# Attention and feed-forward kernel: phi made by GpSimd alone, low parts of weights on VectorE, a new order of all engines

## The chip, the cores and the metric

The kernel runs on one core of one Trainium2 chip. The metric is the device time of one execution in microseconds, as the median of several runs. The engines of the core are called as the profile calls them: PE (TensorE; PEld are its weight loads), DVE (VectorE), ACT (ScalarE), POOL (GpSimd) and SP (SyncE, which here only issues DMAs).

## What is computed

There are 4 batches of 8 heads, 576 positions and head size 64. For each head

```python
scores = q @ k.T / 8, masked causally; a = softmax(scores); local = a @ v
phi(x) = where(x > 0, x, exp(x) - 1) + 1
mem_out = (phi(q) @ M_prev) / (phi(q) @ z_prev + 1e-6)
g = sigmoid(beta)                      # one per head
attn = g * mem_out + (1 - g) * local   # rows: 4 * 576 tokens, 512 columns
h = attn @ w_in1; y = where(h > 0, h, exp(min(h, 0)) - 1) @ w_out1
h = y @ w_in2;    out = (h * clip(h + 3, 0, 6) / 6) @ w_out2
```

The two layers have 512 inputs, 2048 hidden values and 512 outputs. All is float32. Note that phi(x) = max(x, 0) + exp(min(x, 0)), and also max(x + 1, min(exp(x), 1)).

## The kernel before

**Numbers in two parts.** Products that need float32 precision are made from a rounded part (fp32r, named hi) and the rest (lo): x times w is x_hi w_hi + x_hi w_lo + x_lo w_hi. So each tile is rounded by one engine and its low part is made as a subtraction by another.

**Attention.** Two heads form a pair, and there are 16 pairs, handled as a software pipeline: in each step every engine works on two or three pairs in a fixed order that is written out by hand. Queries are cut into four tiles of 128 rows (0 to 3) and a last tile of 64 rows that holds both heads (4). Score tiles are made in the order 4, 3, 2, 1, 0, in two PSUM places in turn, so that `scores` of one tile waits for the exps (`exp_done`) of the tile two before. DVE takes the row maximum (`max_rows`, L951, L955), and ACT the exp with its row sum (`exp_last`, `exp_rows`). PE then transposes the probabilities in chunks (`turn`: G, C00, C01, C10, C11, C2, C3), and also a small tile of row factors R and phi in two pieces (PHI, TAIL). All chunks go through a ring of two PSUM banks, which the product for the first 128 rows (Q0, made by `first_rows`) shares. A chunk is rounded by ACT (`round_chunk`, L731 to L750), its low part made by DVE (`split_chunk`, L962 to L976), and only then is its bank free for the chunk two places on. `first_values` and `times_v` multiply the chunks with v, `times_m` multiplies phi with M, ACT copies one half of the result aside (`low_rows`, `low_first`), and DVE adds the halves into x_all (`sum_x` L1005, `sum_first` L1012).

**phi and the factors.** GpSimd writes x + 1 into the tile phi (`phi_line`, L404), ACT writes exp(x) (`exp_q`, L758), and DVE joins the two (`phi_of_q`, L984). GpSimd multiplies phi with z (`phi_by_z`, L376), DVE sums this (`norms`, L989) and, after the last exp of the pair, makes the reciprocals of all denominators (`row_stats`, L994 to L999). GpSimd makes the row factors from them (`factors`, L386 to L390), scales phi (`scale_phi`, L396), and also scales q (L344), rounds v and M (`round_vm`) and makes their low parts (`low_vm`, L359, L360). The factors of the softmax are turned by PE, sent to DRAM by SP and read back spread over all partitions into r_rows (`spread_r`, L277 to L285), with which GpSimd multiplies the finished pair in x_all (`store_x`, L368).

**Queue of SP.** It issues in order and waits in order: for each step the spread of R, then (in three steps) two weight loads, then the loads of qk and nat (v, q, z and M of a pair) three pairs ahead. nat is released by `low_vm`, phi and `phi_by_z` of two pairs before.

**Feed-forward.** The 2304 tokens are six chunks of 384. A chunk takes 16 hidden tiles: `hidden` (L578, 12 matmuls) and two tiles later `output` (L591, 12 matmuls in the first layer; L599, 9 in the second). Between them, in the first layer, ACT makes the exp (L790) and DVE four operations (L1029, L1031, L1042, L1044); in the second, DVE makes five (L1035 to L1044). Weights come in 32 tiles of 128x1024, through four staging places: DMA, rounding by ACT (`hi_weights`, L695), low part by GpSimd (`lo_weights`, L339); `hidden` waits for this (`w_split`). Tiles 0 to 2 are made during attention. From tile 6 on the place of a tile lies over attention's buffers, so ACT waits for the last `store_x`. The first three groups `hidden` of chunk 0 are woven into the work of the last pair. Tiles of the second layer are made while the last chunk of the first runs, as their places become free, the last four after it.

## Time and profile before

| what | value |
|---|---|
| median of 3 runs | 1075.93 us (1075.89 to 1076.37) |
| the profiled execution, its own time | 1078.44 us |
| its span, first to last instruction | 1076.6 us |
| busy PE / PEld / DVE / ACT / POOL | 1037.4 / 921.7 / 696.7 / 306.1 / 228.5 us |
| mean granted clock of PE | 0.993 |
| moved by DMA | 49.34 MB, 46 GB/s |

The span has four parts. Attention runs from the start to about 258 us, the first layer's work begins at 258.42, the second layer's at about 668, and the rows of the last chunk are stored at the end. Matmuls overlap and their ends are modelled, so a busy share of PE says how long something was under way on it, not how much it could still take. A wait is put down to the instruction that released it last.

### The profile page before, as it was taken

What the parts mean: (1) busy time and instruction counts of PE and PEld (TensorE: products, weight loads), DVE (VectorE), ACT (ScalarE), POOL (GpSimd) and SP (SyncE); (2) the same over time, 40 slices, a digit from 0 to 9 for tenths busy, and PEclk for the clock granted to TensorE, in tenths of its full rate; (3) what the DMA queues carried; (4) which work ended last, traced back from release to release, by engine and by line L of the source; (5) the groups of instructions that cost most, each with busy time, mean ns of one, the idle gap of its engine ahead of it and who ended that gap; (6) DMA issues with size and microseconds to landing.
All of it is one profiled execution on the core that took longest, in us unless ns stands there. A gap on an engine that the chain in (4) does not pass through costs nothing.

```text
span 1076.6 us, 15983 instructions
## 1 busy us (share of the span) xinstructions
PE 1037.4 (96%) x5792; PEld 921.7 (86%) x5792; DVE 696.7 (65%) x1309; ACT 306.1 (28%) x737; POOL 228.5 (21%) x265
## 2 busy tenths in 40 slices
PE   6899999999899999999999999999999999999998
PEld 2666666667899999999999999899899999999997
DVE  4889888988975445454444587756556565565654
ACT  4877777777322121121211234001010010100100
POOL 4676565654640000000000055200000000000000
PEclk8999999999999999999999999999999999999999
DMA  6233532321330000000000033000000000000000
GB/s 235 96 109 117 167 125 98 117 76 40 124 114 1 1 1 0 0 0 0 0 0 0 0 124 109 1 1 30 0 22 7 0 29 0 29 0 0 29 0 30
DMA packets 22007, 49.34 MB, mean 46 GB/s; under 512 B 5184, under 2 KB 5328, under 8 KB 21968
## 3 DMA queue, kind: packets, MB, share of 16 engines
q1 hardware_dynamic: 21968, 48.85, 13.3%
q8 instruction: 21, 0.34, 0.1%
q14 instruction: 18, 0.15, 0.0%
HBM read 44.04 MB, written 4.79 MB: 45 GB/s over the span
## 4 chain that ended last, share of the span: by engine, by line
PE 79%; DVE 16%; ACT 3%; issue 1%; DMA 0%; POOL 0%; ACTq 0%; DVEq 0%
PE ps L578 36%; PE ps L599 19%; PE ps L591 18%; DVE phi L984 3%; DVE neg_max L955 2%; DVE pt_lo L965 2%; DVE x_all L1005 2%; PE ps L464 1%; DVE pt_lo L968 1%; PE ps L519 1%; DVE phi_t_lo L974 1%; PE ps L534 1%; DVE neg_max L951 1%; ACT pt_hi L744 1%; ACT phi_t_hi L748 1%
## 5 line engine op out<-in xcount | busy, mean ns | idle before, releaser
L578 PE MATMUL ps<-x_hi,w 128*128 128x384 f32 x1536 | 391.2, 335 | 0.0
L578 PEld LDWEIGHTS ps<-x_hi,w 128*128 128x128 f32 x1536 | 279.2, 188 | 7.3
L578 PE MATMUL ps<-x_lo,w 128*128 128x384 f32 x768 | 257.7, 336 | 0.0
L591 PE MATMUL ps<-h_hi,w 128*128 128x384 f32 x768 | 196.4, 336 | 4.9 <-DVE h_lo L1044 4.9
L599 PE MATMUL ps<-w,h_hi 128*128 128x512 f32 x576 | 180.3, 394 | 2.1 <-DVE h_lo L1044 2.1
L1042 DVE CAST h_hi<-act_tmp 128x384 fp32r<-128x384 f32 x192 | 109.1, 568 | 101.3 <-PE ps L591 52.5
L339 POOL TENSOR_TENSOR w<-stage,w 128x1024 f32 (+1 forms) x32 | 77.8, 2441 | 345.6 <-ACT w L695 345.6
L591 PEld LDWEIGHTS ps<-h_hi,w 128*128 128x128 f32 x768 | 139.3, 189 | 6.0 <-DVE h_lo L1044 5.9
L578 PEld LDWEIGHTS ps<-x_lo,w 128*128 128x128 f32 x768 | 144.1, 188 | 0.0
L790 ACT ACTIVATE e_act<-ps 128x384 f32<-128x384 f32 x96 | 47.3, 492 | 289.2 <-PE ps L578 289.2
L591 PE MATMUL ps<-h_lo,w 128*128 128x384 f32 x384 | 128.8, 336 | 0.0
L599 PEld LDWEIGHTS ps<-w,h_hi 128*128 128x128 f32 x576 | 107.6, 189 | 20.9 <-issue 2.4
L1044 DVE TENSOR_TENSOR h_lo<-act_tmp,h_hi 128x384 fp32r<-128x384 f32 x192 | 113.4, 591 | 6.7
L1035 DVE TENSOR_SCALAR act_tmp<-ps 128x384 f32<-128x384 f32 x96 | 53.4, 556 | 98.9 <-PE ps L578 98.9
L599 PE MATMUL ps<-w,h_lo 128*128 128x512 f32 x288 | 114.2, 397 | 0.0
L1029 DVE TENSOR_SCALAR act_tmp<-e_act 128x384 f32<-128x384 f32 x96 | 39.6, 413 | 112.7 <-ACT e_act L790 111.3
L767 ACT ACTIVATE x_hi<-x_all 128x384 fp32r (+1 forms) x48 | 21.2, 514 | 300.2 <-PE ps L578 300.2
L591 PEld LDWEIGHTS ps<-h_lo,w 128*128 128x128 f32 x384 | 72.6, 189 | 0.0
L712 ACT ACTIVATE prob<-ps,neg_max 128x512 f32<-128x512 f32 (+3 forms) x128 | 67.0, 526 | 10.7 <-DVE neg_max L955 10.2
L599 PEld LDWEIGHTS ps<-w,h_lo 128*128 128x128 f32 x288 | 54.4, 189 | 11.7
L464 PE MATMUL ps<-qk 64*128 64x512 f32 (+3 forms) x256 | 54.5, 504 | 4.8 <-ACT prob L712 4.8
L1039 DVE TENSOR_TENSOR act_tmp<-ps,act_tmp 128x384 f32<-128x384 f32 x96 | 53.5, 558 | 3.3
(117 smaller groups left out, 1167.7 us busy)
## 6 DMA issues: line engine op xcount, KB each, us to landing
nat<-nat_in SPq DMA_DIRECT2D x16, 768.0 KB, 6.3
qk<-qk_t SPq DMA_DIRECT2D x16, 608.0 KB, 3.9
stage<-w_in SPq DMA_DIRECT2D x32, 256.0 KB, 2.6
stage<-w_out SPq DMA_DIRECT2D x32, 256.0 KB, 2.9
out<-rows_out SPq DMA_DIRECT2D x18, 256.0 KB, 2.1
r_rows<-r_dram SPq DMA_DIRECT2D x32, 128.0 KB, 2.6
r_rows<-r_dram SPq DMA_DIRECT2D x32, 16.0 KB, 2.5
r_dram<-r_turned SPq DMA_DIRECT2D x16, 4.5 KB
```

Source lines behind the costliest of these rows:

```text
L339: pool.tensor_tensor(tile[:, 1], stage[:, r], tile.bitcast(F32)[:, 0], ALU.subtract).then_inc(w_split, 1)
L464: pe.matmul(ps[:, at:at + WIDTH[i]], qk[d, u, P * i:P * i + P], qk[d, u, QCOLS:QCOLS + WIDTH[i]], start=True, stop=False)
L578: mm = pe.matmul(ps[:, bank:bank + CHUNK], w[:, n, wp, 0, cols], xp[:, m, :], start=(m == 0 and part == 0), stop=(m == KM - 1 and part == 2))
L591: mm = pe.matmul(ps[:, Y_AT + 512 * m:Y_AT + 512 * m + CHUNK], w[:, n, wp, 1, cols], hp[:, n % 2, :], start=(n == 0 and part == 0), stop=( ...
L599: mm = pe.matmul(ps[:, Y_AT + 512 * m:Y_AT + 512 * m + DM], hp[:, n % 2, rows], w[:, n, wp, 1, :], start=(n == 0 and part == 0), stop=(n = ...
L712: act.activation(rows_of(u, i, a), ps[:, at:at + WIDTH[i]], ACT.Exp, bias=neg_max[:, u, x:x + 1], scale=-1.0, accum_out=stats[:, u, x:x + ...
L790: act.activation(e_act[:, n % 2, :], ps[:, 512 * (n % 4):512 * (n % 4) + CHUNK], ACT.Exp).then_inc(h_exp_done, 1)
L1029: dve.tensor_scalar(tmp, e_act[:, n % 2, :], 1.0, -1.0, ALU.min, ALU.add).then_inc(e_free, 1)
L1035: dve.tensor_scalar(tmp, h, 3.0, 0.0, ALU.add, ALU.max).then_inc(act_step, 1)
L1039: dve.tensor_tensor(tmp, h, tmp, ALU.mult).then_inc(h_free, 1)
L1042: dve.tensor_copy(h_hi[:, n % 2, :], tmp).then_inc(h_hi_done, 1)
L1044: dve.tensor_tensor(h_lo[:, n % 2, :], tmp, h_hi.bitcast(F32)[:, n % 2, :], ALU.subtract).then_inc(h_split, 1)
```

## The change

Six things change together.

1. phi is now max(x, 0) + exp(min(x, 0)). GpSimd makes min(x, 0) (`cut_q`), ACT its exp in place (`exp_q`), GpSimd max(x, 0) (`phi_line`) and the sum (`phi_sum`). DVE's `phi_of_q` is gone.
2. r_rows has two buffers, each with a semaphore of its own.
3. Weight tiles 3 to 31 get their low part from DVE, one after each tile of activations, in chunk 0 of the first layer, in its last chunk (from hidden tile 5), and in the first chunk of the second layer (the last five). Tiles 0 to 2 stay on GpSimd. DVE's loops over chunks are cut so that these chunks stand outside.
4. SP issues the first four weight loads one step at a time, behind nat, and the next three two steps apart.
5. ACT's rounding of weights 0 to 2 moves to steps 5 to 7, at the end of the step.
6. The order inside a step is new. With A the pair whose chunks are turned and B and C the next two, it is now:

- PE: C11, C2 of A; scores 1 of B; C3, times_v 1, PHI, times_v 2 of A; scores 0 of B; TAIL, times_v 3 and 4 of A; G of B; times_m of A; scores 4 of C; first_rows of A; C00 of B; scores 3 of C; C01, C10 of B; scores 2 of C; first_values 0, R, first_values 1 of B.
- ACT: exps 3 (head 0) of B; R of A; exps 3 (head 1) of B; C11, C2 of A; exps 2 (head 0) of B; C3 of A; exps 2 (head 1) and 1 (head 0) of B; PHI, TAIL of A; exps 1 (head 1) and 0 of B; G of B; low_rows, low_first of A; C00 of B; exp_q of C; exp_last of C; C01, C10 of B.
- DVE: row_stats, G of A; sum_x of the pair before A; maximum 4 of B; sum_first of the pair before A; C00 of A; maximum 3 of B; C01, C10 of A; maximum 2 of B; C11, C2 of A; maximum 1 of B; C3, PHI of A; maximum 0 of B; TAIL of A; (gates in the first step); norms of B.
- POOL: phi_by_z, round_vm of A; scale_q, cut_q, phi_line of B; factors, low_vm of A; store_x two pairs before A; scale_phi of A; (a weight in three steps); phi_sum of B.

Before, PE issued scores 0 after G and scores 1 after C11; DVE made row_stats after maximum 3, G and the sums at the step's end. The diff, without these order lists of PE, ACT and DVE:

```diff
...
-    r_rows = sb("r_rows", [S])
+    r_rows = sb("r_rows", [2, S])
-    r_loaded = semaphore("r_loaded")
+    r_loaded = [semaphore(f"r_loaded{i}") for i in range(2)]
-    phi_relu_done = semaphore("phi_relu_done")
+    q_cut = semaphore("q_cut")
+    phi_line_done = semaphore("phi_line_done")
...
             def load_nat(p):
                 if p >= 2:
                     sp.wait_ge(vm_split, p - 1)
-                    sp.wait_ge(phi_done, p - 1)
                     sp.wait_ge(phi_z_done, p - 1)
                 sp.dma_start(nat[:, p % 2, :], nat_in[p]).then_inc(nat_loaded[p % 2], 16)
             def spread_r(p):
+                if p >= 2:
+                    sp.wait_ge(r_loaded[p % 2], 64 * (p // 2))
                 sp.wait_ge(rounded[R], p + 1)
                 sp.dma_start(r_dram[p % 2], r_turned[0:2 * FULL + 1, :]).then_inc(r_sent, 16)
                 sp.wait_ge(r_sent, 16 * (p + 1))
-                if p >= 1:
-                    sp.wait_ge(x_stored, p)
+                if p >= 2:
+                    sp.wait_ge(x_stored, p - 1)
                 for a in range(2):
                     main = r_dram[p % 2, FULL * a:FULL * a + FULL].rearrange("i q -> (i q)").rearrange("(o x) -> o x", o=1)
                     tail = r_dram[p % 2, 2 * FULL:2 * FULL + 1, REST * a:REST * a + REST]
-                    sp.dma_start(r_rows[D * a:D * a + D, 0:EDGE], main.to_broadcast([D, EDGE])).then_inc(r_loaded, 16)
-                    sp.dma_start(r_rows[D * a:D * a + D, EDGE:S], tail.to_broadcast([D, REST])).then_inc(r_loaded, 16)
+                    sp.dma_start(r_rows[D * a:D * a + D, p % 2, 0:EDGE], main.to_broadcast([D, EDGE])).then_inc(r_loaded[p % 2], 16)
+                    sp.dma_start(r_rows[D * a:D * a + D, p % 2, EDGE:S], tail.to_broadcast([D, REST])).then_inc(r_loaded[p % 2], 16)
             load_qk(0)
             load_nat(0)
             sp.dma_start(beta_sb[:, :], beta.to_broadcast([P, H])).then_inc(beta_loaded, 16)
             load_qk(1)
             load_nat(1)
-            for n in range(STAGES):
-                sp.dma_start(stage[:, n, 0, :], w_in1[n]).then_inc(w_loaded[n], 16)
-                sp.dma_start(stage[:, n, 1, :], w_out1[n]).then_inc(w_loaded[n], 16)
             def load_weights(n):
-                sp.wait_ge(w_split, n - STAGES + 1)
+                if n >= STAGES:
+                    sp.wait_ge(w_split, n - STAGES + 1)
                 sp.dma_start(stage[:, n % STAGES, 0, :], w_in1[n]).then_inc(w_loaded[n % STAGES], 16)
                 sp.dma_start(stage[:, n % STAGES, 1, :], w_out1[n]).then_inc(w_loaded[n % STAGES], 16)
             for g in range(3, PAIRS + 4):
                 if is_pair(g - 4):
                     spread_r(g - 4)
-                if 9 <= g < 9 + EARLY:
-                    load_weights(g - 9 + STAGES)
+                if g in (9, 11, 13):
+                    load_weights(STAGES + (g - 9) // 2)
                 if is_pair(g - 1):
                     load_qk(g - 1)
                     load_nat(g - 1)
+                if 3 <= g < 3 + STAGES:
+                    load_weights(g - 3)
...
-            def lo_weights(tile, n, r):
+            def lo_weights(n):
                 pool.wait_ge(w_hi_done, n + 1)
-                pool.tensor_tensor(tile[:, 1], stage[:, r], tile.bitcast(F32)[:, 0], ALU.subtract).then_inc(w_split, 1)
...
                 x = x_all[:, at:at + S]
                 pool.wait_ge(x_summed, p + 1)
                 pool.wait_ge(q0_summed, p + 1)
-                pool.wait_ge(r_loaded, 64 * (p + 1))
-                pool.tensor_tensor(x, x, r_rows[:, :], ALU.mult).then_inc(x_stored, 1)
+                pool.wait_ge(r_loaded[p % 2], 64 * (p // 2 + 1))
+                pool.tensor_tensor(x, x, r_rows[:, p % 2, :], ALU.mult).then_inc(x_stored, 1)
...
+            def cut_q(p):
+                u = p % 2
+                pool.wait_ge(nat_loaded[u], 16 * (p // 2 + 1))
+                q = nat[:, u, QT * P:2 * QT * P].rearrange("p (t c) -> p t c", t=QT)
+                pool.tensor_scalar(phi_exp[:, :, :], q, 0.0, 1.0, ALU.min, ALU.mult).then_inc(q_cut, 1)
             def phi_line(p):
                 u = p % 2
-                pool.wait_ge(nat_loaded[u], 16 * (p // 2 + 1))
                 if p >= 2:
                     pool.wait_ge(turned[TAIL], p - 1)
                 q = nat[:, u, QT * P:2 * QT * P].rearrange("p (t c) -> p t c", t=QT)
-                pool.tensor_scalar(phi[:, u], q, 1.0, 1.0, ALU.add, ALU.mult).then_inc(phi_relu_done, 1)
+                pool.tensor_scalar(phi[:, u], q, 0.0, 1.0, ALU.max, ALU.mult).then_inc(phi_line_done, 1)
+            def phi_sum(p):
+                u = p % 2
+                pool.wait_ge(phi_line_done, p + 1)
+                pool.wait_ge(phi_exp_done, p + 1)
+                pool.tensor_tensor(phi[:, u], phi[:, u], phi_exp[:, :, :], ALU.add).then_inc(phi_done, 1)
             scale_q(0)
             pool.memset(prob[:, :, P_ALL - D:P_ALL], 0.0).then_inc(zeros_ready, 1)
-            for g in range(2, PAIRS + 3):
-                if is_pair(g - 6):
-                    store_x(g - 6)
-                if is_pair(g - 5):
-                    scale_phi(g - 5)
-                if is_pair(g - 3):
-                    phi_line(g - 3)
-                if is_pair(g - 4):
-                    low_vm(g - 4)
+            for g in range(2, PAIRS + 2):
                 if is_pair(g - 3):
                     phi_by_z(g - 3)
-                if 5 <= g < 5 + EARLY:
-                    lo_weights(w[:, g - 5], g - 5, g - 5)
+                    round_vm(g - 3)
                 if is_pair(g - 2) and g >= 3:
                     scale_q(g - 2)
-                if is_pair(g - 3):
-                    round_vm(g - 3)
-                if is_pair(g - 4):
-                    factors(g - 4)
-            scale_phi(PAIRS - 2)
+                if is_pair(g - 2):
+                    cut_q(g - 2)
+                    phi_line(g - 2)
+                if is_pair(g - 3):
+                    factors(g - 3)
+                    low_vm(g - 3)
+                if is_pair(g - 5):
+                    store_x(g - 5)
+                if is_pair(g - 3):
+                    scale_phi(g - 3)
+                if g in (7, 9, 11):
+                    lo_weights((g - 7) // 2)
+                if is_pair(g - 2):
+                    phi_sum(g - 2)
+            phi_by_z(PAIRS - 1)
+            round_vm(PAIRS - 1)
             low_vm(PAIRS - 1)
-            store_x(PAIRS - 3)
             factors(PAIRS - 1)
             scale_phi(PAIRS - 1)
-            lo_weights(w[:, EARLY], EARLY, EARLY)
+            store_x(PAIRS - 3)
             store_x(PAIRS - 2)
             store_x(PAIRS - 1)
-            with pool.Fori(1, KF // STAGES) as g:
-                for r in range(STAGES):
...
-                u = p % 2
-                act.wait_ge(nat_loaded[u], 16 * (p // 2 + 1))
-                if p >= 1:
-                    act.wait_ge(phi_done, p)
-                act.activation(phi_exp[:, :, :], nat[:, u, QT * P:2 * QT * P].rearrange("p (t c) -> p t c", t=QT), ACT.Exp).then_inc(phi_exp_done, 1)
+                act.wait_ge(q_cut, p + 1)
+                act.activation(phi_exp[:, :, :], phi_exp[:, :, :], ACT.Exp).then_inc(phi_exp_done, 1)
             def x_round(c, phase):
...
-            def phi_of_q(p):
-                u = p % 2
-                dve.wait_ge(phi_relu_done, p + 1)
-                dve.wait_ge(phi_exp_done, p + 1)
-                dve.scalar_tensor_tensor(out=phi[:, u], in0=phi_exp[:, :, :], scalar=1.0, in1=phi[:, u], op0=ALU.min, op1=ALU.max).then_inc(phi_done, 1)
...
+            def lo_weights(n):
+                dve.wait_ge(w_hi_done, n + 1)
+                dve.tensor_tensor(w[:, n % KF, 1], stage[:, n % STAGES], w.bitcast(F32)[:, n % KF, 0], ALU.subtract).then_inc(w_split, 1)
...
+            lo_weights(EARLY)
             for n in range(1, KF):
                 activate(0, n, 0)
-            for phase in range(2):
-                with dve.Fori(1 - phase, CHUNKS) as c:
-                    x_rest(c, phase)
-                    for n in range(KF):
-                        activate(c, n, phase)
+                if n + EARLY < KF:
+                    lo_weights(n + EARLY)
+            with dve.Fori(1, CHUNKS - 1) as c:
+                x_rest(c, 0)
+                for n in range(KF):
+                    activate(c, n, 0)
+            x_rest(CHUNKS - 1, 0)
+            for n in range(KF):
+                activate(CHUNKS - 1, n, 0)
+                if n >= 5:
+                    lo_weights(KF + n - 5)
+            x_rest(0, 1)
+            for n in range(KF):
+                activate(0, n, 1)
+                if n < 5:
+                    lo_weights(2 * KF - 5 + n)
+            with dve.Fori(1, CHUNKS) as c:
+                x_rest(c, 1)
+                for n in range(KF):
+                    activate(c, n, 1)
```

## Rows read from the trace of the kernel before

**Rows 1.** Windows: stretch, its length, busy us of each engine, granted clock, DMA, GB/s
```profile
258.42:327.92 69.50, 65.45 (x372) 64.11 (x370) 54.87 (x68) 21.55 (x32) 34.75 (x15) 0.98 0.32 104
327.92:660.72 332.80, 332.80 (x1922) 332.80 (x1921) 174.70 (x339) 66.64 (x131) 26.43 (x11) 1.00 0.05 16
660.72:732.63 71.91, 68.99 (x347) 62.88 (x346) 48.39 (x85) 8.51 (x14) 12.44 (x5) 0.98 0.05 15
732.63:1066.90 334.27, 334.27 (x1681) 303.27 (x1681) 200.40 (x420) 17.80 (x35) 0.00 (x0) 1.00 0.03 12
```

**Rows 2.** Timeline: start, us, engine, line; maximum of tile 2, score tile 2
```profile
15.23 1.55 DVE L955 TENSOR_REDUCE neg_max<-ps 128x2 f32<-128x768 f32 x2
...
25.37 0.92 PE L464 MATMUL ps<-qk 64*128 64x384 f32 x4
...
240.89 0.92 PE L464 MATMUL ps<-qk 64*128 64x384 f32 x4
```

**Rows 3.** Chain that ended last, one pair (118 to 134): start, us, work
```profile
126.96 1.98 DVE phi L984
...
129.88 0.67 DVE neg_max L951
...
130.57 0.62 DVE x_all L1005
...
132.15 0.28 DVE x_all L1012
```

**Rows 4.** Windows: one whole pair, and PE from times_m to C01 within it
```profile
118.00:133.34 15.34, 14.21 (x93) 9.63 (x94) 13.63 (x25) 11.62 (x33) 9.15 (x15) 1.00 0.45 143
127.98:131.74 3.76, 3.76 (x25) 2.52 (x23) 3.72 (x6) 3.17 (x8) 1.83 (x2) 1.00 0.89 295
```

**Rows 5.** Waits of PE's weight loads in this pair: us, times, longest
```profile
PEld ps L503 <- DVE x_all L1012: 0.8, 1, 0.8
...
PEld ps L534 <- DVE pt_lo L965: 0.7, 1, 0.7
...
PEld ps L503 <- DVE pt_lo L965: 0.6, 2, 0.3
...
PEld ps L519 <- DVE pt_lo L968: 0.6, 1, 0.6
```

**Rows 6.** Line L984: durations min/median/max in ns, first and last start
```profile
L984 DVE SCALAR_TENSOR_TENSOR phi<-phi_exp,phi x16: 824/2060/2073, 14.5 to 234.1; 128x640 f32<-128x640 f32 x16
```

**Rows 7.** Timeline: GpSimd's operation beside L984
```profile
126.71 1.55 POOL L360 TENSOR_TENSOR v_split<-nat,v_split 128x640 fp32r<-128x640 f32 x1
```

**Rows 8.** Groups by line and shape, GpSimd in this pair: busy us, mean ns
```profile
L376 POOL TENSOR_TENSOR phi_z<-phi,nat 128x640 f32<-128x640 f32 x1 | 1.6, 1550 | 0.8 <-DVE phi L984 0.8
...
L404 POOL TENSOR_SCALAR phi<-nat 128x640 f32<-128x640 f32 x1 | 0.7, 723 | 2.3 <-PE ps L521 2.3
```

**Rows 9.** Waits of GpSimd in this pair
```profile
POOL phi L404 <- PE ps L521: 2.3, 1, 2.3
POOL r_nat L386 <- DVE inv L999: 1.6, 1, 1.6
POOL qk L344 <- DMA qk<-qk_t: 1.4, 1, 1.4
```

**Rows 10.** Timeline of the hand-over to the first layer
```profile
269.80 12.70 POOL L339 TENSOR_TENSOR w<-stage,w 128x1024 f32 x5
...
270.09 2.62 DVE L1044 TENSOR_TENSOR h_lo<-act_tmp,h_hi 128x384 fp32r<-128x384 f32 x1
```

**Rows 11.** Windows: the stretches behind PE's longest wait in each hand-over
```profile
280.33:284.24 3.91, 3.91 (x13) 3.91 (x14) 3.81 (x5) 0.00 (x0) 2.17 (x1) 0.56 0.57 166
...
676.40:680.40 4.00, 4.00 (x11) 3.24 (x12) 3.90 (x4) 0.00 (x0) 4.00 (x2) 0.58 0.00 0
```

**Rows 12.** Group of DVE's low parts of x in undisturbed chunks: busy us, mean ns
```profile
L1019 DVE TENSOR_TENSOR x_lo<-x_all,x_hi 128x384 fp32r<-128x384 f32 x20 | 9.8, 552 | 0.1
```

**Rows 13.** DMA issues of the page: count, KB each, median us to landing
```profile
nat<-nat_in SPq DMA_DIRECT2D x16, 768.0 KB, 6.3
```

More of the change, by code:

```diff
@@ L605, in _ @@
             pe.wait_ge(masks_ready, 1)
[L606 removed]
+            for g in range(1, PAIRS + 1):
                 if is_pair(g - 3):
[L608 to L628 removed]
                     turn(g - 3, C11)
+                    turn(g - 3, C2)
                 if is_pair(g - 2):
@@ L641, in _ @@
                     times_v(g - 3, 4)
-            last = PAIRS - 1
+                if is_pair(g - 2):
+                    turn(g - 2, G)
+                if is_pair(g - 3):
+                    times_m(g - 3)
+                if is_pair(g - 1):
+                    scores(g - 1, 4)
+                if is_pair(g - 3):
+                    first_rows(g - 3)
+                if is_pair(g - 2):
+                    turn(g - 2, C00)
+                if is_pair(g - 1):
+                    scores(g - 1, 3)
+                if is_pair(g - 2):
+                    turn(g - 2, C01)
+                    turn(g - 2, C10)
+                if is_pair(g - 1):
+                    scores(g - 1, 2)
+                if is_pair(g - 2):
+                    first_values(g - 2, 0)
+                    turn(g - 2, R)
+                    first_values(g - 2, 1)
+            last = PAIRS - 1
+            turn(last - 1, C11)
+            turn(last - 1, C2)
+            scores(last, 1)
+            turn(last - 1, C3)
+            times_v(last - 1, 1)
+            turn(last - 1, PHI)
+            times_v(last - 1, 2)
+            scores(last, 0)
+            turn(last - 1, TAIL)
+            times_v(last - 1, 3)
+            times_v(last - 1, 4)
             turn(last, G)
-            scores(last, 0)
             times_m(last - 1)
@@ new lines, in _ @@
+                if is_pair(g - 2):
+                    exp_rows(g - 2, 1, 1)
+                    exp_rows(g - 2, 0, 0)
+                    exp_rows(g - 2, 0, 1)
+                    round_chunk(g - 2, G)
+                if is_pair(g - 3):
+                    low_rows(g - 3)
+                    low_first(g - 3)
+                if is_pair(g - 2):
+                    round_chunk(g - 2, C00)
+                if is_pair(g - 1):
+                    exp_q(g - 1)
+                    exp_last(g - 1)
@@ L852, in _ @@
+                if is_pair(g - 2):
+                    round_chunk(g - 2, C01)
+                    round_chunk(g - 2, C10)
+                if 5 <= g < 5 + EARLY:
+                    hi_weights(g - 5)
             last = PAIRS - 1
+            exp_rows(last, 3, 0)
+            round_chunk(last - 1, R)
+            exp_rows(last, 3, 1)
+            round_chunk(last - 1, C11)
             round_chunk(last - 1, C2)
+            exp_rows(last, 2, 0)
             round_chunk(last - 1, C3)
             exp_rows(last, 2, 1)
+            exp_rows(last, 1, 0)
@@ L1091, in _ @@
             split_chunk(last, C00)
-            row_stats(last)
             split_chunk(last, C01)
```

124 lines of the change are left out of this document (37 added, 87 removed).

## The prediction

> **What bounds the kernel now.** I read the busy times by stretch first, since shares of the whole span (PE, that is TensorE, 96%) mix stages [rows 1]. From 327.92 to 660.72 us and from 732.63 to 1066.90 PE is busy without a gap: this is the feed-forward part, and it has no slack to give. Three stretches can move: attention, its hand-over to the first layer (258.42 to 327.92), and the hand-over to the second (660.72 to 732.63).
>
> In attention the third score tile of a pair starts at 25.37 us for pair 1 and at 240.89 for pair 15 [rows 2]: (240.89 - 25.37) / 14 = 15.39 us a pair, and 15.34 in the pair that I read closely. The chain of waits through that pair [rows 3] runs mostly over VectorE (DVE): phi itself (L984, 1.98 us, once a pair), row maxima, the sums into x_all, and then PE's next transpose, which waits for them. Busy in this pair: PE 14.21, DVE 13.63, ScalarE (ACT) 11.62, GpSimd (POOL) 9.15 [rows 4]. So DVE's order bounds the pair, with PE close behind. PE is idle for 15.34 - 14.21 = 1.1 us by its busy time, but its modelled ends reach into waits; its weight loads wait 0.8 + 0.7 + 0.6 + 0.6 = 2.7 us for DVE [rows 5]. I take the middle, 1.9: PE's own work is about 15.34 - 1.9 = 13.5 us (ends: 12.6 and 14.2).
>
> L984 needs 0.82 us when GpSimd is idle (its minimum) and takes 2.06 at the median [rows 6]. GpSimd's L360 begins at 126.71 and lasts 1.55, so ends at 128.26 [rows 7]; L984, ready at 126.9, ends at 128.94 [rows 3], which is 128.26 plus 0.68. It stands still while GpSimd works. The same shows where GpSimd makes low parts of weights: a subtraction on 384 columns that takes 0.55 us elsewhere [rows 12] takes 2.62 in the first hand-over, beside a row of five such GpSimd operations of 12.70 / 5 = 2.5 us [rows 10].
>
> **The change, part by part.** The sum is made against the profiled execution: span 1076.6, its own time 1078.44, against a median of 1075.93. I take the difference over to the median.
>
> *phi.* DVE loses L984, 2.06 us a pair. GpSimd keeps the line operation (0.72, now a maximum) and gains cut_q, the same form, 0.72, and phi_sum, with two inputs of 128x640: between 0.72 (one input) and 1.55 (L376, two) [rows 8]. I take 1.55, the row of its own form. GpSimd goes from 9.15 to 9.15 + 0.72 + 1.55 = 11.4 us a pair, below 13.5: that is the cover. Without it the 2.27 us come once a pair. ACT's exp only reads another tile; it waits for cut_q, behind which stand the exps of tile 4 and C01's rounding on ACT; cut_q runs about half a pair ahead of it.
>
> In the Trainium skill, "GPSIMD Engine Reference", section 4.1, says that elementwise work belongs on VectorE, GpSimd being about twice as slow with two inputs. The trace agrees: 1.55 against 0.82 [rows 6, 8]. By that rule alone each pair would lose 2.27 - 0.82 = 1.45 us wherever both lie on the path. Against it stands "SBUF — State Buffer", section "Who interferes with whom": a DVE operation with two SBUF inputs and a GpSimd operation that reads SBUF shut each other out for a whole instruction. By this rule, which [rows 3, 7] fit, DVE wins the full 2.06.
>
> *Order.* Taking 1.98 out of a chain of 15.34 leaves 13.4, just below PE's 13.5, so PE and the round trips decide. I followed one pair through the new order. Between the end of times_m and transpose C01, PE has 3.76 us of work (score tile 4, first_rows, C00, score tile 3) [rows 4]. C01 needs sum_first: ACT copies x_low, about 1.1, then DVE does sum_x 2 x 0.62, a maximum 0.67, sum_first 2 x 0.28 [rows 3]: 3.6 in all. Just in time, where PE's loads now wait 0.8 [rows 5]. Score tile 2 needs the exp of tile 4, behind which ACT now also has exp_q (0.75): about 0.4 of wait. R, C11 and C3 wait for splits by about 0.15 together. Score tile 0, issued before TAIL, brings row_stats about 2 us earlier, so that factors and low_vm on GpSimd (about 3 us) end some 2.5 us before first_values wants them. A pair is then 13.5 + 0.55 = 14.05 us. Ends: 13.5 (no wait left) and 15.34 (a chain of the present length forms anew). Over 14 pairs: 14 x (15.39 - 14.05) = 18.8 us; ends 26.5 and 0.
>
> *Start.* Now ACT's exp of pair 0, the gates and phi stand on DVE ahead of the maximum of tile 2, at 15.23 [rows 2]. In the new order it follows the first maximum, near 11.4; gates and norms come after all maxima of pair 0. Tile 1's exps end near 15.4, row_stats and the split of G near 19.0, and score tile 2 of pair 1 starts near 22.1 in place of 25.37 [rows 2]: 3.3 us; ends 0 and 3.8.
>
> *Row factors in two buffers, and the DMA queue.* Inside attention r_rows is wanted two pairs after it is made, so its extra buffer buys nothing there. For the last pair its loads no longer wait for the store before; but that store waits for x_summed too, which comes late: counted as 0. It is hidden by the eight groups of PE work before weight 6 is wanted; uncovered it could cost what the hand-over now loses, 6.5. In SP's queue weight loads now stand behind nat, not ahead of it. The load of nat is released by low_vm, and cut_q waits for it, and the next low_vm for that: 6.3 us to landing [rows 13] and about 4.5 of GpSimd work, 11 us in a period of 14. This ring stays slack; at a landing of 9.5 it would bind.
>
> *Low parts of weights on DVE.* 29 of 32 move. 384 columns take 0.55 us [rows 12] and 448 take 0.62 [rows 3], 1.1 ns a column, so 1024 take 0.55 + 640 x 1.1 ns = 1.25 us; the upper end is GpSimd's 2.5. DVE is busy 174.7 of 332.8 us in 80 steps of the first layer [rows 1], 2.2 of 4.16 a step; 3.45 with a weight is covered, 4.7 at the upper end is not and would cost 28 x 0.5 = 14 us. What goes is GpSimd's hold on DVE.
> First hand-over: a group of 12 matmuls is 332.8 / 160 = 2.08 us; 69.5 us less 29 groups (60.3) less the end of the last pair (a fifth of 13.5, 2.7) leaves 6.5 us lost: PE waiting for h_lo, and after that wait a stretch at a granted clock of 0.56, mostly at 1.2 GHz [rows 11]. The last stores by GpSimd still meet the first weights: 1.0 stays. Gain 5.5; ends 2 and 6.5. Second hand-over: a chunk of layer two takes 334.27 / 5 = 66.85, this one 71.91: 5.06 lost, again with a stretch at 0.58 [rows 1, 11]. DVE now meets nothing of GpSimd there. Gain 5.0; ends 3 and 5.06.
>
> Sum: 18.8 + 3.3 + 5.5 + 5.0 = 32.6 us. The profiled execution comes to about 1045.8, the median to 1075.93 - 32.6 = 1043.3, so 1043.
>
> **Rivals.** *A: PE's floor is reached,* the round trips cost nothing. For it: the waits that I leave are tenths of a us. 26.5 + 3.5 + 5.5 + 5.0 = 40.5: 1035. *B: the chain forms anew* over ACT and DVE. For it: ACT is busy 11.6 us in a strict order, with exp_q and the exp of tile 4 now ahead of C01. Against it: the 1.98 us taken away lie on the chain itself. A pair stays at 15.39, the ends gain 3.3 + 10.5 = 13.8: 1062. *C, slower: GpSimd becomes the bound.* It waits 2.3 us for TAIL, 1.6 for inv and 1.4 for qk [rows 9]. If its single order keeps all three beside 11.4 of work, a pair takes 16.7: scaled phi and low_vm come late and hold PE. That is 14 x 1.3 = 18 us lost, the start too, 10.5 won: 1083. It decides from a pair of 15.39 + 10.5 / 14 = 16.1 us. Against it: TAIL and qk are asked for later in its order, when they are long there. The first page named above speaks for C. *D: the weights cost DVE 2.5 us each,* and row_stats is caught behind GpSimd, a pair taking 14.6: 11.1 + 3.3 + 10.5 - 14 = 10.9: 1065.
>
> **Chances.** Forecast (1038 to 1052) 0.61; A 0.1; B 0.13; D 0.05; C 0.09; about no change 0.02. Less than 0.2% (2.2 us) can't be told from no change. Faster: 0.61 + 0.1 + 0.13 + 0.05 = 0.89; same 0.02; slower 0.09. The range takes in A and B: 1034 to 1063.
>
> **What would show it.** From score tile 2 to score tile 2 near 14.05 us; no DVE row in attention stretched by GpSimd, which is busy about 11.4 a pair; subtractions of 0.55 at both hand-overs, no stretch near a clock of 0.56, the second hand-over 66.9 us long; low parts at 1.25 us on DVE. I am wrong if the period stays above 15, if GpSimd waits for nothing in a pair (C), or if PE's first-layer groups wait for low parts of weights (D).

## The result, and the profile after

The kernel after takes 1060.78 us (median, 1060.32 to 1061.26), the kernel before beside it 1076.15; the ratio is 0.985, with an interval of 0.984 to 0.987. Forecast were 1043 us (1038 to 1052), a gain of 32.9; the gain is 15.4. The number lies close to the 1062 of rival B, whose mechanism, as e1 below shows, is not the cause. The profiled execution has 1060.6 us and a span of 1058.8.

The page after, busy times, slices and the chain that ended last:

```profile
PE 1031.7 (97%) x5792; PEld 924.2 (87%) x5792; DVE 656.0 (62%) x1322; ACT 300.4 (28%) x737; POOL 244.9 (23%) x268
...
POOL 8999999995000000000000000000000000000000
...
PE 83%; POOL 11%; DVE 3%; issue 1%; ACT 1%; DMA 1%; POOLq 0%; SPq 0%; DVEq 0%
```

The same line of the page before:

```profile
PE 79%; DVE 16%; ACT 3%; issue 1%; DMA 0%; POOL 0%; ACTq 0%; DVEq 0%
```

GpSimd is busy in nine tenths and more of nearly every slice of attention, and it is now 11% of the chain, where DVE had 16%. The forecast had named this sign: "if GpSimd waits for nothing in a pair (C)". Its operations in five pairs (150 to 225 us; busy, mean ns, idle before):

```profile
L405 POOL TENSOR_SCALAR phi_exp<-nat 128x640 f32<-128x640 f32 x5 | 11.8, 2358 | 0.0
L412 POOL TENSOR_SCALAR phi<-nat 128x640 f32<-128x640 f32 x5 | 11.8, 2358 | 0.0
L418 POOL TENSOR_TENSOR phi<-phi,phi_exp 128x640 f32<-128x640 f32 x6 | 9.4, 1559 | 0.0
```

cut_q (L405) and phi_line (L412) take 2.36 us each, where L404 of before, one input, the same tile, took 0.72 [rows 8]. phi_sum (L418) takes 1.56 as forecast. Here are two stretches, from one cut_q to the next: one with a low part of a weight on GpSimd (2.4 us) and a plain one (length, busy PE, PEld, DVE, ACT, POOL, granted clock, DMA share, GB/s). The third row spans 14 pairs, from the third score tile of pair 1 to that of pair 15:

```profile
104.88:122.08 17.20, 14.29 (x96) 9.85 (x96) 12.75 (x26) 12.72 (x35) 17.04 (x18) 1.00 0.52 165
168.99:183.86 14.87, 14.87 (x106) 10.80 (x106) 12.96 (x27) 12.51 (x40) 14.71 (x17) 1.00 0.47 155
24.86:233.88 209.02, 197.34 (x1289) 138.86 (x1288) 166.53 (x323) 159.24 (x452) 206.82 (x222) 0.97 0.40 130
```

GpSimd's own work is the period: 14.7 busy in 14.87, and 206.8 in the 209.0 of 14 pairs. A step with a weight takes it 17.2, so the three low parts that stayed on GpSimd add 7 us, which the forecast's sum for GpSimd did not hold. PE does not follow evenly. Its early pairs take 13.5 to 13.9, with GpSimd's first steps at 13.5 too, and two later ones 19.3 and 18.6, with a granted clock of 0.82; GpSimd is busy in 19.2 and 18.5 of these two, so it is not the clock that sets them. A piece of the chain of waits in the first stretch is GpSimd's work alone:

```profile
104.23 0.70 POOL qk L346
104.92 2.32 POOL phi_exp L405
107.24 2.32 POOL phi L412
...
112.41 1.38 POOL x_all L370
113.79 1.22 POOL phi L398
115.00 2.36 POOL w L341
117.36 1.50 POOL phi L418
```

The third score tile of pair 1 and of pair 15, the counterpart of [rows 2]:

```profile
24.86 0.59 PE L473 MATMUL ps<-qk 64*128 64x384 f32 x2
...
233.88 0.59 PE L473 MATMUL ps<-qk 64*128 64x384 f32 x2
```

So the start won 25.37 - 24.86 = 0.5 us, and 14 pairs took 209.0 instead of 215.5: 6.5 us, 14.93 a pair on average. The rest of the gain lies behind attention. Two of the stretches of [rows 1] are now, in the same columns:

```profile
315.39:648.18 332.79, 332.79 (x1921) 332.79 (x1921) 167.74 (x350) 66.62 (x131) 0.00 (x0) 1.00 0.04 14
648.18:715.09 66.91, 66.91 (x347) 61.80 (x346) 46.11 (x90) 8.63 (x14) 0.00 (x0) 1.00 0.08 24
```

The second hand-over takes 66.91 in place of 71.91 (5.0), at a clock of 1.00. From pair 15's third score tile to the end of the first hand-over it was 327.92 - 240.89 = 87.03 and is 315.39 - 233.88 = 81.51 (5.5). Together 0.5 + 6.5 + 5.5 + 5.0 = 17.5, which agrees with the spans (1076.6 - 1058.8 = 17.8). The medians differ by 15.4, since the profiled execution of before lies 2.3 us above the 1076.15 (2.5 above the 1075.93 from which the forecast starts) and the one of after 0.2 below its own; so what is read here as a difference of two traces may be up to that much too large in the medians.

### The profile page after: what moved, and what is told of

Same layout as the page of the kernel before. It is cut to its first block, busy times and chain, and to the rows that moved or that the text cites. A ratio compares the mean times of both kernels' runs of the same rounds, so it can differ in the third digit from the quotient of the medians.

```text
span 1058.8 us, 15807 instructions
## 1 busy us (share of the span) xinstructions
PE 1031.7 (97%) x5792; PEld 924.2 (87%) x5792; DVE 656.0 (62%) x1322; ACT 300.4 (28%) x737; POOL 244.9 (23%) x268
## 3 DMA queue, kind: packets, MB, share of 16 engines
q1 hardware_dynamic: 21968, 48.85, 13.9%
## 4 chain that ended last, share of the span: by engine, by line
PE 83%; POOL 11%; DVE 3%; issue 1%; ACT 1%; DMA 1%; POOLq 0%; SPq 0%; DVEq 0%
PE ps L587 38%; PE ps L600 19%; PE ps L608 19%; POOL phi_exp L405 2%; PE ps L473 2%; POOL phi L412 2%; POOL phi_z L378 1%; POOL phi L418 1%; PE ps L552 1%; POOL v_split L362 1%; PE ps L512 1%; POOL phi L398 1%; DVE x_all L1015 1%; POOL x_all L370 1%; POOL w L341 1%
## 5 line engine op out<-in xcount | busy, mean ns | idle before, releaser
L1057 DVE CAST h_hi<-act_tmp 128x384 fp32r<-128x384 f32 x192 | 69.1, 360 | 101.2 <-PE ps L600 54.5
L1059 DVE TENSOR_TENSOR h_lo<-act_tmp,h_hi 128x384 fp32r<-128x384 f32 x192 | 107.2, 559 | 6.7
L1044 DVE TENSOR_SCALAR act_tmp<-e_act 128x384 f32<-128x384 f32 x96 | 35.7, 372 | 119.0 <-ACT e_act L808 117.6
L972 DVE TENSOR_REDUCE neg_max<-ps 128x2 f32<-128x1024 f32 (+1 forms) x64 | 52.2, 815 | 6.9 <-PE ps L476 6.8
L1046 DVE SCALAR_TENSOR_TENSOR act_tmp<-ps,act_tmp 128x384 f32<-128x384 f32 x96 | 53.5, 558 | 3.3
```

What stands on the lines that cost most here:

```text
L972: dve.tensor_reduce(neg_max[:, u, 2 * i:2 * i + 2], rows, AX_X, ALU.min).then_inc(max_done[i], 1)
L1044: dve.tensor_scalar(tmp, e_act[:, n % 2, :], 1.0, -1.0, ALU.min, ALU.add).then_inc(e_free, 1)
L1046: dve.scalar_tensor_tensor(out=tmp, in0=h, scalar=0.0, in1=tmp, op0=ALU.max, op1=ALU.add).then_inc(h_free, 1)
L1057: dve.tensor_copy(h_hi[:, n % 2, :], tmp).then_inc(h_hi_done, 1)
L1059: dve.tensor_tensor(h_lo[:, n % 2, :], tmp, h_hi.bitcast(F32)[:, n % 2, :], ALU.subtract).then_inc(h_split, 1)
```

## The experiments

The theory to be tested: min and max are slow forms on GpSimd, they alone make it the bound, and every other term holds. The rivals: the two operations are slow because something shares their port or their tiles; the scalar 0.0 in them makes them slow; or the chain over DVE and ACT binds anyway (rival B).

**e2_forms: one form after another,** on GpSimd at the end of the kernel, while no other engine works (the eleven forms; o is another stretch of x_all each time):

```
pool.tensor_scalar(o, a, 1.0, 1.0, ALU.add, ALU.mult)    # L460; L461 min, mult; L462 max, mult
pool.tensor_scalar(o, a, 1.0, 0.0, ALU.mult, ALU.max)    # L463; L464 mult, add; L465 max alone
pool.tensor_tensor(o, a, b, ALU.add)                     # L466; L467 subtract
                                                         # L468: L461 on 320 columns
pool.tensor_scalar(o, a, 0.0, 1.0, ALU.subtract, ALU.mult)  # L469; L470 copy
```

> The changed kernel with ten operations of GpSimd behind all other work, while every other engine is idle, each on 128x640 float32 in SBUF: add-mult, min-mult, max-mult, mult-max, mult-add, max alone, two inputs added, two inputs subtracted, min-mult on 320 columns, subtract-mult, and a copy. Theory P: what costs is min or max itself, with no other engine near: 2.36 us for min-mult, max-mult and mult-max, 0.72 for add-mult and mult-add, about 1.2 for min-mult on 320 columns, 1.55 for two inputs. Rival L (a lock, or reading the tile q beside ACT and DVE, makes it slow in attention): all one-input forms take 0.72 here. Rival Z (the scalar 0.0 makes the slow form): mult-add with 0.0 and subtract-mult with 0.0 are slow too.

Its timeline on GpSimd (start, duration):

```profile
1059.14 2.35 POOL L461 TENSOR_SCALAR x_all<-x_all 128x640 f32<-128x640 f32 x1
1061.46 2.35 POOL L462 TENSOR_SCALAR x_all<-x_all 128x640 f32<-128x640 f32 x1
1063.78 2.36 POOL L463 TENSOR_SCALAR x_all<-x_all 128x640 f32<-128x640 f32 x1
1066.11 0.72 POOL L464 TENSOR_SCALAR x_all<-x_all 128x640 f32<-128x640 f32 x1
1066.80 1.82 POOL L465 TENSOR_SCALAR x_all<-x_all 128x640 f32<-128x640 f32 x1
1068.58 1.53 POOL L466 TENSOR_TENSOR x_all<-x_all 128x640 f32<-128x640 f32 x1
1070.07 1.53 POOL L467 TENSOR_TENSOR x_all<-x_all 128x640 f32<-128x640 f32 x1
1071.57 1.29 POOL L468 TENSOR_SCALAR x_all<-x_all 128x320 f32<-128x320 f32 x1
1072.83 2.35 POOL L469 TENSOR_SCALAR x_all<-x_all 128x640 f32<-128x640 f32 x1
1075.13 0.72 POOL L470 COPY x_all<-x_all 128x640 f32<-128x640 f32 x1
```

The form decides, with nothing beside it: min, max and also subtract in this instruction take 2.35 us, add with mult and mult with add 0.72 (L460 too). That something shared slows them falls as a cause, and so does the scalar 0.0, which mult with add has as well. The price grows with the columns: it is 1.29 for half of them. An operation with two inputs is cheaper (1.53) than a min on one.

**e1_add, e8_one_add, e9_line_sub: the cheap form in place of both, of one, and another exact form.**

```diff
# e1 and e8
-pool.tensor_scalar(phi_exp[:, :, :], q, 0.0, 1.0, ALU.min, ALU.mult).then_inc(q_cut, 1)
+pool.tensor_scalar(phi_exp[:, :, :], q, 0.0, 1.0, ALU.add, ALU.mult).then_inc(q_cut, 1)
...
# e1 too
-pool.tensor_scalar(phi[:, u], q, 0.0, 1.0, ALU.max, ALU.mult).then_inc(phi_line_done, 1)
+pool.tensor_scalar(phi[:, u], q, 0.0, 1.0, ALU.add, ALU.mult).then_inc(phi_line_done, 1)
...
# e9 alone: x - min(x, 0), for which ACT's exp in place now waits
-pool.tensor_scalar(phi[:, u], q, 0.0, 1.0, ALU.max, ALU.mult).then_inc(phi_line_done, 1)
+pool.tensor_tensor(phi[:, u], q, phi_exp[:, :, :], ALU.subtract).then_inc(phi_line_done, 1)
```

> The changed kernel with one thing different: the two one-input operations on GpSimd, min(q, 0) and max(q, 0), are q + 0 instead (same shapes, waits and places), so phi is computed wrongly. Theory P (price of min and max on GpSimd): each falls from 2.36 to 0.72 us, GpSimd's work per pair from 14.87 to 11.6, below PE's own 13.5, so the pair is set by PE and its round trips: period of score tile 2 near 14.05 (13.5 to 14.4), time about 1060.8 - 14 x 0.88 = 1048 (1041 to 1052). Rival R (the chain over ACT and DVE formed anew near 14.9 by itself, GpSimd only keeps step with it): GpSimd becomes idle for 3 us a pair, the period stays at 14.8 to 14.9, time 1059 to 1061.

> The changed kernel with only min(q, 0) replaced by q + 0 (phi is wrong); max(q, 0) stays. GpSimd's work per pair is 14.87 - 1.64 = 13.2 us. Theory G (the slower of GpSimd's sum and PE's 13.5 sets the pair): 13.2 is under 13.5, so nearly all of the gain of replacing both is there: period 13.5, in the three pairs with a weight on GpSimd 15.6, and 1041 to 1043 (both replaced: 1039.2). Rival P2 (each us taken from GpSimd's queue counts by itself, half the work gives half the gain): 1050.

> The changed kernel with max(q, 0) made as q - min(q, 0), a subtraction of two tiles (1.55 us in place of 2.36), with ACT's exp in place waiting for it. GpSimd's sum per pair is 14.87 - 0.81 = 14.06. Theory G: period 14.06, time 1060.8 - 0.81 x 14 = 1049.5 (1048 to 1051). A rival by which a two-input operation costs more in place, through locks with DVE, gives 1053 or more.

e1 takes 1039.2 us (ratio 0.965, 0.964 to 0.967), e8 1042.5 (0.968, 0.966 to 0.970), e9 1053.2 (0.978, 0.976 to 0.980). In e1 and e8 phi is another function, so they measure time alone. One pair of e1 and of e9, same columns as above:

```profile
119.72:133.23 13.51, 13.51 (x93) 9.61 (x93) 11.62 (x24) 11.14 (x33) 11.86 (x18) 1.00 0.52 176
```

```profile
169.00:183.15 14.15, 13.80 (x94) 9.68 (x92) 12.00 (x24) 11.17 (x33) 13.91 (x17) 1.00 0.42 146
```

In e1 PE has no gap in the whole pair: its floor of 13.5 is reached, below the 14.05 that I had forecast, and the time is below the range expected for e1 (1041 to 1052). Rival B falls with it: order and chain are those of the kernel after, and the pair does not stay near 14.9. In e8, as expected, with 13.1 us of work on GpSimd, 11 of 14 pairs take 13.5 to 13.9. In e9, with 13.9 of work, the last pairs take 14.15; after, with 14.7, they take 14.87. So GpSimd costs little up to PE's 13.5 and from there on about its excess. For e9 I had expected 1049.5 (1048 to 1051), a saving of 0.8 us on GpSimd in each of 14 pairs, and missed. Its time lies where the rival expected it, but not by the rival's cause: the subtraction takes 1.54 us in place, no more than alone. GpSimd did lose 11.6 us of work in these pairs, but stood idle for 6.7 of them in place of 2.2, and pair 1's third score tile came 0.9 us later. The early pairs ran at 13.5 to 13.9 in the kernel after already and had little to win.

**e4_weights: the kernel before with only the weights' low parts on DVE,** tiles 3 to 31, by the loops of the change; attention is untouched.

```diff
+            def lo_weights(n):          # on DVE, after an activate(...)
+                dve.wait_ge(w_hi_done, n + 1)
+                dve.tensor_tensor(w[:, n % KF, 1], stage[:, n % STAGES], w.bitcast(F32)[:, n % KF, 0], ALU.subtract).then_inc(w_split, 1)
```

> The kernel before with one part of the change: the low parts of weights 3 to 31 come from DVE, in the places where the change has them; phi, order and row factors stay. Theory H (the two hand-overs are a matter of their own, lost to GpSimd's hold on DVE): 5.0 us at the second hand-over and 5.5 at the first, 1076.2 - 10.5 = 1065.7; the attention period stays 15.39. Rival (the first hand-over was won by the new order of the last pair or by the earlier store): only 5 to 6 us in all, 1070 to 1071.

1068.3 us (ratio 0.992, 0.990 to 0.994). The two hand-overs, from pair 15's third score tile and at the second layer:

```profile
241.04:322.78 81.74, 79.76 (x479) 74.64 (x479) 62.40 (x114) 36.05 (x72) 11.49 (x17) 1.00 0.29 92
655.58:722.49 66.91, 66.91 (x346) 61.80 (x346) 46.11 (x90) 8.63 (x14) 0.00 (x0) 1.00 0.08 24
```

They take 81.74 against 87.03 and 66.91 against 71.91: 5.3 and 5.0 us in the traces, by this edit alone, with the period of a pair at 15.32 as before. In medians it is 7.6 us, between what the theory (10.5) and its rival (5 to 6) expected; the profiled execution of before, 2.5 us above its median, would fill the difference. What GpSimd's low parts held up on DVE was more than the subtractions of [rows 10]. The rounding into h_hi, with one input, took 1.65 us on average where GpSimd made them and takes 0.36 now, as everywhere else. Here it is at the end of the first layer, before and in e4:

```profile
L1042 DVE CAST h_hi<-act_tmp 128x384 fp32r<-128x384 f32 x14 | 23.0, 1645 | 7.0 <-PE ps L591 6.9
```

```profile
L1039 DVE CAST h_hi<-act_tmp 128x384 fp32r<-128x384 f32 x11 | 4.0, 360 | 7.1 <-PE ps L583 7.1
```

**e14_phi_cheap, e12_phi_only: the kernel before with only phi moved,** the cheap and the true form. Order, weights and buffers stay.

```diff
                 if is_pair(g - 3):
+                    cut_q(g - 3)
                     phi_line(g - 3)
                 if is_pair(g - 4):
                     low_vm(g - 4)
                 if is_pair(g - 3):
+                    phi_sum(g - 3)
                     phi_by_z(g - 3)
...
-                if is_pair(g - 1):
-                    phi_of_q(g - 1)        # DVE
```

> e12_phi_only with add in place of min and max (phi is another function then, so the output differs). GpSimd has 0.72 twice, 11.4 us a pair. Theory, the prediction's step of DVE's chain: 1.98 us leave the chain of 15.34 and a pair takes 13.5 to 14.1: 1054 (1050 to 1060). Rival: the old order's round trips form the chain anew, a pair keeps 14.6 or more: 1065 or more.

> The kernel before with only phi changed as in the change (min, exp in place, max, sum on GpSimd, nothing on DVE): the order, the weights and the buffers stay. GpSimd's work is then 9.15 - 0.72 + 2 x 2.36 + 1.55 = 14.7 us a pair; the minimum lies in its idle 2.3 us before TAIL. Theory: GpSimd holds the period at 14.9 to 15.2 us, DVE's 2 us buy nearly nothing, and the time is 1072 (1069 to 1076). Rival: GpSimd's strict order leaves some of its waits beside 14.7 of work, a pair takes 15.5 to 16.5 and the time is 1079 to 1092.

e14 takes 1072.7 us (ratio 0.997, 0.996 to 0.998), e12 1084.3 (1.006, 1.005 to 1.008). My theory missed in both, and both lie where the rivals expected them. One pair of e14, and then of e12:

```profile
141.90:156.73 14.83, 14.21 (x95) 9.60 (x94) 11.79 (x23) 11.62 (x33) 11.80 (x17) 1.00 0.40 134
```

```profile
189.73:204.58 14.85, 14.20 (x92) 9.60 (x92) 11.82 (x24) 11.65 (x32) 14.69 (x17) 1.00 0.36 116
```

DVE has 1.8 us less work than in [rows 4], but the period falls only from 15.32 to 14.83. The chain of waits of e14 shows what took the place:

```profile
143.77 0.76 DVE neg_max L963
...
144.56 0.62 DVE x_all L1011
...
145.84 0.28 DVE x_all L1018
...
146.47 0.67 DVE pt_lo L977
147.14 1.13 DVE neg_max L967
...
148.70 0.28 DVE inv L1005
148.98 0.56 DVE pt_lo L977
149.58 0.67 PE ps L549 x2
```

From 143.77 to 149.53 DVE works on the chain without a pause: a maximum that must wait for score tile 4, the four sums that stand behind it (L1011 and L1018 twice each, one row of each shown), two splits, a maximum and the reciprocals, and only then PE goes on. In the old order taking out L984 only starts this piece earlier by what other waits allow. Its 1.98 us were on the chain; of them 0.5 were worth anything. e12 adds the slow forms: the last six pairs take 14.84 to 14.93, since 14.7 of work on GpSimd just fit, and the four before them at 15.3. But its first pairs take up to 19.3 us, those with a weight's low part (17.0 of work on GpSimd) above all. The longest of them has a granted clock of 0.82, so a part of its length is PE's own work at a lower clock.

**e7_join_early, e10_best, e13_one_r: the new order with phi made as before.** GpSimd writes x + 1, ACT exp(x), and DVE joins them right behind the maximum of score tile 2. Weights and the two buffers of row factors are those of the change.

```diff
...
-                pool.tensor_scalar(phi[:, u], q, 0.0, 1.0, ALU.max, ALU.mult).then_inc(phi_line_done, 1)
+                pool.tensor_scalar(phi[:, u], q, 1.0, 1.0, ALU.add, ALU.mult).then_inc(phi_line_done, 1)
...
                 if is_pair(g - 2):
-                    cut_q(g - 2)
                     phi_line(g - 2)
...
-                if is_pair(g - 2):
-                    phi_sum(g - 2)
...
                 if is_pair(g - 2):
                     max_rows(g - 2, 2)
+                    phi_of_q(g - 2)          # DVE
```

> As the kernel with the old phi in the new order (1135.6), but DVE joins phi right after the maximum of tile 2, half a pair earlier, so that GpSimd finds it done. Theory Q (that kernel lost 60 us to the place: GpSimd stood 8.8 us a pair at phi_by_z with scale_q, and so PE's next scores, queued behind it): DVE has 11.6 + 0.8 to 2.1 us a pair, GpSimd 9.3, the period falls from 20.5 to 13.6 to 14.2, time 1041 to 1050. Rival M (a join on DVE costs in any place, since GpSimd shuts it out for 1.2 us and the round trips of PE run through DVE): 15 us or more, 1060 or more.

e7 takes 1042.5 us (ratio 0.969, 0.966 to 0.971). A pair of it, and its joins (min/median/max ns):

```profile
149.17:162.77 13.60, 13.55 (x94) 9.61 (x93) 12.26 (x25) 11.16 (x33) 9.30 (x15) 1.00 0.51 162
...
L1002 DVE SCALAR_TENSOR_TENSOR phi<-phi_exp,phi x16: 814/814/1590, 11.8 to 219.6; 128x640 f32<-128x640 f32 x16
```

This is the finding of the study: with phi where it was, 18 us faster than the kernel after. The join takes 0.81 us, not 2.06 [rows 6], because in this order GpSimd waits for it (`phi_by_z`, 2.2 us a pair) and so stands idle while it runs. DVE's work of 12.3 us fits into 13.6. Only in the three steps with a weight on GpSimd did the two meet (1.58 to 1.59); those pairs take 14.4.

e10 moves that weight's operation into GpSimd's idle time before phi_line, e13 gives e7 a single buffer of row factors:

```diff
                     scale_q(g - 2)
+                if g in (7, 9, 11):           # e10; stood at the end of the step
+                    lo_weights((g - 7) // 2)
...
-    r_rows = sb("r_rows", [2, S])             # e13
+    r_rows = sb("r_rows", [1, S])
-                if p >= 2:
-                    sp.wait_ge(x_stored, p - 1)
+                if p >= 1:
+                    sp.wait_ge(x_stored, p)
```

> e7_join_early (new order, GpSimd x+1 with add, ACT exp of q, DVE's join right after the maximum of tile 2) with one move more: in the three steps in which GpSimd makes the low part of a weight (2.38 us) it does so between scale_q and phi_line, where it is idle for 0.55 + 1.33 us, and not after scale_phi, where it shut out DVE's join (1.59 instead of 0.81 us) and made those steps 14.4 us instead of 13.6. Theory (GpSimd's operation holds DVE only where both meet): the three steps come to 13.5 to 13.8 and the time to 1040.5 (1039.3 to 1042). Rival: the operation now makes phi_line, factors and scaled phi late by 0.5 us each time and the steps stay at 14.4 or more: 1042.5 to 1044.

> e7_join_early with one buffer of row factors in place of two, as in the kernel before. Prediction's step: the second buffer was counted as 0. Theory N: 0 holds; the loads of the factors of a pair wait for the store of the pair before, some 11 us more in SP's queue, and behind them stand qk and nat, wanted about 6 us after that: just in time. 1042.5 (1042 to 1043.5). Rival S: the queue's wait makes qk and nat late by up to 0.7 us a pair, GpSimd waits for DMA before scale_q or phi_line, and the time is 1045 to 1053.

e10 takes 1041.9 us (ratio 0.968, 0.967 to 0.969), inside the expected range. But only one of the three steps came to 13.6 us as expected, the other two to 14.2. The interval overlaps that of e7: whether the move gains anything isn't settled.

e13 takes 1056.4 (ratio 0.982, 0.980 to 0.983), 14 us more than e7 and more than even its rival expected (1045 to 1053). The waits of SP's queue from 65 to 180 us, of e13 and then of e7 (total, times, longest):

```profile
SPq L283 <- POOL x_all L371: 83.6, 8, 12.2
```

```profile
SPq L273 <- POOL v_split L363: 37.0, 8, 4.8
SPq L279 <- ACT r_turned L751: 29.4, 9, 3.6
```

The queue stands up to 12.2 us before it may load a pair's row factors, and behind them stand, in some steps, a weight tile and then qk and nat of a later pair. Here are such issues on SP (start, duration) and, under them, GpSimd waiting for that qk:

```profile
143.98 0.58 SPq L298 DMA_DIRECT2D stage<-w_in  x1
...
145.09 0.43 SPq L266 DMA_DIRECT2D qk<-qk_t  x1
...
151.75 0.73 POOL L347 TENSOR_SCALAR qk<-qk 128x640 f32<-128x640 f32 x1 [3.66 <-DMA qk<-qk_t]
```

Three steps of e13 take 17.3, 21.1 and 16.6 us; the other steps keep to 13.5 to 14.8. In the last two a weight's load was issued ahead of qk and qk came 3.7 us late. In the first GpSimd made a weight's low part, but so it did in a step of 14.6, so what made this one long isn't shown. In all three the granted clock fell too, to 0.90, 0.76 and 0.90, and PE's busy time rose from 13.5 to 15.4, 17.5 and 15.1: a part of the 14 us is PE's own work at a lower clock, behind the waits. The kernel before has one buffer as well. Its queue waits for R itself, and hardly for the store:

```profile
SPq L277 <- ACT r_turned L731: 56.4, 7, 8.1
...
SPq L280 <- POOL x_all L368: 2.9, 7, 0.4
```

There R is made late in the step, shortly before that store ends. The new order makes R early, and by that makes the second buffer necessary.

**e6_relu_act: phi without min and max, and off DVE.** ACT makes n = relu(-x), then exp(-n); GpSimd adds x + n and then the sum. ACT's two stand between low_rows and low_first, GpSimd's two at the end of its step.

```diff
+act.activation(phi[:, u], nat[:, u, QT * P:2 * QT * P].rearrange("p (t c) -> p t c", t=QT), ACT.Relu, scale=-1.0).then_inc(q_cut, 1)
...
+act.activation(phi_exp[:, :, :], phi[:, u], ACT.Exp, scale=-1.0).then_inc(phi_exp_done, 1)
...
+pool.tensor_tensor(phi[:, u], q, phi[:, u], ALU.add).then_inc(phi_line_done, 1)
```

> A version that keeps phi exact without min or max on GpSimd: ACT makes n = relu(-q) (0.74) and exp(-n), both between low_rows and low_first, where it waits for PE; GpSimd makes q + n and the sum, 2 x 1.55. GpSimd has 14.87 - 4.72 + 1.55 = 11.7 us a pair, ACT 11.1 + 0.75. Theory G: PE's 13.5 sets the pair, time 1038 to 1041, as with both operations cheap (1039.2). Rival: ACT's two operations delay low_first and with it C01, a wait of 0.3 to 0.7 us a pair, 1044 to 1050.

1042.9 us (ratio 0.969, 0.967 to 0.971), between what theory (1038 to 1041) and rival (1044 to 1050) expected. Most pairs take 13.5, those with a weight on GpSimd 14.4. It keeps the thought of the change, nothing of phi on DVE, and is as fast as e7 within their intervals.

**e5_old_phi: as e7, but the join late on DVE, before norms.**

```diff
+                if is_pair(g - 2):
+                    phi_of_q(g - 2)          # DVE, behind split TAIL
                     norms(g - 2)
```

> The changed kernel with phi made as before: GpSimd q + 1, ACT exp of q, DVE joins the two by min and max, behind the low part of TAIL and ahead of norms; new order, two r_rows and weights on DVE stay. It tells what the order does without the move of phi. GpSimd has 9.9 us a pair or less. Theory O (the new order is most of what attention won): DVE's operation costs 0.8 to 2.1 us but the round trips are shorter, period 14.2 to 14.9, time 1050 to 1060. Rival M (the move of phi is what won, the order nothing): the chain over DVE stays, period about 15.3, time 1065 to 1067.

1135.6 us (ratio 1.055, 1.053 to 1.057), pairs of 20.5: neither theory. Waits from 100 to 233 us, and the window over 14 pairs:

```profile
POOL phi_z L379 <- DVE phi L1002: 56.6, 6, 11.2
...
PEld ps L467 <- POOL qk L347: 19.0, 6, 3.2
...
26.99:308.54 281.55, 242.17 (x1289) 169.34 (x1289) 184.91 (x337) 160.28 (x452) 134.15 (x198) 0.77 0.28 95
```

GpSimd's phi_by_z waits up to 11 us for the join, and scale_q, which stands behind it, makes PE's next score tile late by up to 3.2 us, and the rest of the step with it. The granted clock over these 14 pairs is 0.77, where e7 has 1.00, and PE is busy 242 us in place of 191: the waits make a gap, and PE's work itself takes longer too. Both together, the place of one operation of 0.8 us is worth 93 us here; what it would cost at the full clock isn't shown.

## Why the prediction was wrong, step by step

- **The step that failed**: "cut_q, the same form, 0.72", and the "line operation (0.72, now a maximum)". I took L404's duration for another operation of the same instruction and the same tile. Both take 2.36. GpSimd's sum of 11.4 us a pair was 14.7 (17.0 in the three steps with a weight, which the sum had left out), the "cover" of 13.5 was gone, and the pair took 14.93 in place of 14.05. By its sign this is rival C, GpSimd the bound in a strict order, but with its price from work, not from waits: it loses against PE's 13.5, and still wins against the old 15.39. With the cheap form (e1) the kernel comes to 1039.2: these two operations cost 21.6 us, more than the 17.5 by which the forecast missed; so other terms were off the other way.
- **PE's floor**, 13.5 of work a pair: right (e1: 13.51). Of the 0.55 us of round trips on top of it 0.1 were there, since e1's 14 pairs take 13.61 on average, those with a weight's low part on GpSimd included; rival A was right there.
- **The chain over DVE.** "Against it: the 1.98 us taken away lie on the chain itself" was wrong as an argument. They did, and e14 shows that the old order forms the chain anew at 14.83; e7 shows that the new order reaches 13.6 with this work still on DVE. I had the wrong part of the change for the cause: the new order, with its second buffer, gives most of attention's gain. No run has the new phi in the new order with one buffer, and none takes the new places of the weight loads and of ACT's rounding (parts 4 and 5 of the change) by themselves, so their share isn't shown.
- **Row factors in two buffers, "counted as 0"**: wrong by 14 us in the new order with the join on DVE (e13 against e7). I asked when r_rows is wanted, and not how long the queue stands before its load and what is behind. The sum was not hurt, as the change has both.
- **The start**, 3.3 forecast, 0.5 measured. e1, with the cheap forms, gets 25.37 - 23.78 = 1.6; so 1.1 belongs to min and max, and the other 1.7 I had overrated.
- **Hand-overs and weights**: 5.5 and 5.0 forecast, 5.5 and 5.0 in the traces, and by e4 they belong to this part. Low parts on DVE took 1.22 us each (forecast 1.25, so rival D with 2.5 is out), and the trace names nobody who waits for them. The 12.70 us of five GpSimd operations, and with them the stretched rows on DVE, are gone. What is open is the absolute size in medians, up to 2.5 us less.
- The profiled execution's 2.5 us over the median I had carried over as it was; the sum of gains read from its trace may have been too large by about that.

The two pages that the forecast weighed can be judged now. The join on DVE took 0.81 us with GpSimd idle. Beside GpSimd's subtraction it took 1.59 and ended 0.68 after it (e7), as in the kernel before, which fits "SBUF — State Buffer", section "Who interferes with whom", of the Trainium skill. But "GPSIMD Engine Reference", section 4.1, of the Trainium skill, by which elementwise work belongs on VectorE, was the better guide to what to do: phi there is 18 us faster (e7 against the kernel after), once the order keeps the two apart.

## What to carry to other kernels

A duration depends on the operation too, not only on engine, instruction, shape and type: before work is moved, time the exact form by itself, and give the receiving engine a total with the upper bound. If the moved work takes a chain away, follow what starts next on the same engine, for here the new order with its second buffer was worth some 26 us (e7 against e4) and the freed 2 us a pair only 3 (e14 against before). A wait that repeats can cost more than its own length: in e5 and e13 the granted clock fell with it. A queue that issues in order makes each buffer a question about everything behind it.
